# Expert tiles with the down product behind the next tile's up product, and all transposes in one place on 64 rows

## The reference

```python
def _moe2_ref(x, w_gate, w_local, w1, w2):          # x 4x576x512, w1 8x512x1024, w2 8x1024x512
    logits = np.einsum('bsd,de->bse', x, w_gate)
    local_gate = 1.0 / (1.0 + np.exp(-np.einsum('bsd,de->bse', x, w_local).squeeze(-1)))
    for b in range(B):
        prev_e = -1
        for s in range(S):
            fresh_e = int(np.argmax(logits[b, s]))
            e = fresh_e if (s == 0 or local_gate[b, s] < 0.5) else (prev_e if prev_e >= 0 else fresh_e)
            prev_e = e
            p = softmax(logits[b, s])
            h = np.maximum(x[b, s] @ w1[e], 0.0)
            out[b, s] = p[e] * (h @ w2[e])
```

## Time and profile before

| | us |
|---|---|
| median of 3 runs | 859.98 |
| lowest and highest | 859.12, 860.97 |
| the profiled execution: its time | 860.46 |
| its span between first and last record | 858.6 |
| PE busy (share of the span) | 841.0 (98%) |

### The profile page before, as it was taken

The page is one execution under the profiler, slowest core; times in us unless marked ns, Lnnn a source line. Parts: engine busy times, 40 slices in busy tenths (PEclk is TensorE's granted clock), DMA queues, the critical chain, the costliest instruction groups (busy, mean ns, idle before and its releaser), DMA issues.

```text
span 858.6 us, 19447 instructions
## 1 busy us (share of the span) xinstructions
PE 841.0 (98%) x7168; PEld 728.8 (85%) x7169; DVE 403.5 (47%) x730; ACT 340.7 (40%) x751; POOL 243.1 (28%) x286
## 2 busy tenths in 40 slices
PE   7899999999999999999999999999999999999996
PEld 6899999799999998799989989988778888888885
DVE  5677777511255245335536754543872432432221
ACT  4677777411145236215513522541432432522221
POOL 5977878793000000000000000039141112112111
PEclk9999999999999999999999999999999999999999
DMA  7454443139222012102201202415341341311111
GB/s 170 133 140 119 113 118 102 52 124 24 11 86 65 13 50 67 31 1 87 62 1 62 62 25 81 165 37 186 125 155 39 128 146 37 132 45 43 37 37 43
DMA packets 36088, 67.68 MB, mean 79 GB/s; under 512 B 11336, under 2 KB 11464, under 8 KB 36040
## 3 DMA queue, kind: packets, MB, share of 16 engines
q1 hardware_dynamic: 26168, 44.90, 19.7%
q10 hardware_dynamic: 6512, 11.64, 4.5%
q0 software_dynamic: 3360, 10.49, 3.8%
HBM read 57.58 MB, written 9.98 MB: 79 GB/s over the span
## 4 chain that ended last, share of the span: by engine, by line
PE 90%; DVE 3%; ACT 2%; POOL 2%; issue 1%; DMA 1%; ACTq 0%; POOLq 0%; DVEq 0%
PE bank L1700 23%; PE bank L1702 23%; PE bank L1701 23%; PE bank L1640 4%; PE bank L1585 4%; PE bank L1610 4%; PE bank L1893 2%; PE bank L1595 1%; PE bank L1747 1%; PE bank L1845 1%; DMA stage<-gate_rows 1%; DVE stage L1173 1%; PE bank L1573 1%; PE bank L1776 1%; PE bank L1626 1%
## 5 line engine op out<-in xcount | busy, mean ns | idle before, releaser
L1142 DVE SCALAR_TENSOR_TENSOR hid_lo<-bank,hid_hi 128x384 fp32r<-128x384 f32 x96 | 53.5, 557 | 210.1 <-ACT hid_hi L971 210.0
L1702 PE MATMUL bank<-uT_hi,W 128*128 128x384 f32 x384 | 129.8, 338 | 0.0
L1700 PE MATMUL bank<-uT_hi,W 128*128 128x384 f32 x384 | 129.6, 338 | 0.0
L1701 PE MATMUL bank<-uT_lo,W 128*128 128x384 f32 x384 | 129.1, 336 | 0.0
L971 ACT ACTIVATE hid_hi<-bank 128x384 fp32r<-128x384 f32 x96 | 46.9, 488 | 186.9 <-PE bank L1702 186.8
L995 ACT ACTIVATE stage<-stage 128x512 f32<-128x512 f32 x135 | 84.6, 627 | 77.0 <-DVE stage L1173 70.5
L1700 PE MATMUL bank<-W,hid_hi 128*128 128x512 f32 x288 | 114.0, 396 | 0.1
L1702 PE MATMUL bank<-W,hid_lo 128*128 128x512 f32 x288 | 113.8, 395 | 0.0
L1701 PE MATMUL bank<-W,hid_hi 128*128 128x512 f32 x288 | 113.6, 394 | 0.0
L1173 DVE TENSOR_TENSOR stage<-rows,stage 128x512 f32<-128x512 f32 x135 | 89.0, 687 | 10.7 <-ACT stage L995 8.5
L1404 DVE TENSOR_TENSOR hT_lo<-bank,hT_hi 128x512 fp32r<-128x512 f32 x40 | 27.6, 691 | 105.5 <-ACT hT_hi L1034 105.5
(11 more groups left out here) (287 smaller groups left out, 1528.9 us busy)
## 6 DMA issues: line engine op xcount, KB each, us to landing
rows<-in_moe_w SPq DMA_DIRECT2D x12, 1024.0 KB, 6.4
stage<-gate_rows ACTq DMA_DIRECT2D x38, 256.0 KB, 3.2
stage<-in_moe_w_ch SPq DMA_DIRECT2D x16, 512.0 KB, 3.8
qk_raw<-in_q SPq DMA_DIRECT2D x32, 144.0 KB, 3.6
vv<-in_v SPq DMA_DIRECT2D x32, 144.0 KB, 2.8
x_rows<-rows SPq DMA_DIRECT2D x6, 768.0 KB, 3.2
qk_raw<-in_k SPq DMA_DIRECT2D x30, 144.0 KB, 3.5
late_stage<-in_moe_w SPq DMA_DIRECT2D x4, 1024.0 KB, 6.6
```

Source lines behind the costliest of these rows:

```text
L1142: dve.scalar_tensor_tensor(out=hid_lo[:, n % 2], in0=bank[:, HB[n % 2], 0:TOK], scalar=0.0, in1=hid_hi[:, n % 2].bitcast(F32), op0=ALU.max ...
L1700: pe.matmul(dst, lhs_hi, rhs_hi, start=start, stop=False)
L1701: pe.matmul(dst, lhs_hi, rhs_lo, start=False, stop=False)
L1702: return pe.matmul(dst, lhs_lo, rhs_hi, start=False, stop=stop)
```

## The change

- **Order on PE.** A step of tile i is now: both up halves of tile i (24 matmuls), the whole down product of tile i - 1 (24 matmuls), then in one place the transposes of h of tile i, both halves, and of x of tile i + 2. The down product of the last tile stands alone behind the loop. In the written-out part the down product of tile 2 is cut: chunks 0 to 3 stand before the loop, 4 to 7 in step 3.
- **Transposes on 64 rows.** Each 128x128 transpose of the loop becomes two of 64 rows by 128 columns, one for each half of the tokens, which write to two banks (2 and 3, or 6 and 7). 24 instead of 12 per tile. In front of each group stands `settled(pe)`, a semaphore count of no other use.
- **A second transposed x.** `xT_hi_odd`, `xT_lo_odd` lie on memory of `rows`; the loop runs over pairs of tiles, even and odd. Tile i + 2 is transposed in step i, and tile i + 3 is gathered behind it; before it was i + 1 and i + 2.
- **ACT and DVE.** Splits of weights (both kinds) stand at the start of a step, ahead of the relus, and before they stood behind a tile's work, but for the case DOWN_NOW. `weigh(i - 1)` comes in step i, ahead of the low parts of h.

```diff
@@ the loop @@
         def expert_steps(eng, step):
             end = load_last(eng)
-            with eng.Fori(EARLY_T + 1, FULL) as i:
-                step(i)
-            with eng.Fori(FULL, TILES) as i:
-                with eng.If(end >= i):
-                    step(i)
+            step(EARLY_T + 1, 1)
+            with eng.Fori(EARLY_T // 2 + 1, FULL // 2) as n:
+                step(2 * n, 0)
+                step(2 * n + 1, 1)
+            with eng.Fori(FULL // 2, TILES // 2) as n:
+                for odd in range(2):
+                    with eng.If(end >= 2 * n + odd):
+                        step(2 * n + odd, odd)
             return end
@@ POOL @@
-            def step(i):
+            def step(i, par):
                 scatter(i - 1)
-                pool.wait_ge(xg_used, i + 2)
-                gather(i + 2)
+                pool.wait_ge(xg_used, i + 3)
+                gather(i + 3)
@@ POOL, before the loop @@
             scatter(0)
+            pool.wait_ge(xg_used, 3)
+            gather(4)
...
             scatter(1)
-            pool.wait_ge(xg_used, 4)
-            gather(4)
+            pool.wait_ge(xg_used, 5)
+            gather(5)
@@ ACT @@
+            def hT_halves(i, g):
+                act.wait_ge(tr_done, 2 * i + g + 1)
+                act.wait_ge(b_done, i)
+                if g == 1:
+                    act.wait_ge(xg_used, i + 3)
+                act.activation(by_half(hT_hi[:, 4 * g:4 * g + 4]), turned_half(g, H_COLS[g]), ACT.Copy)\
+                   .then_inc(hT_hi_out, 1)
-            def step(i):
+            def step(i, par):
                 todo = table(act, TODO, i, 7)
-                with act.If((todo & DOWN_NOW) != 0):
-                    prepare(i - 1, 1)
-                tile_work(i)
-                with act.If((todo & DOWN_LATER) != 0):
+                with act.If((todo & (DOWN_LATER | DOWN_NOW)) != 0):
                     prepare(i - 1, 1)
                 with act.If((todo & UP) != 0):
                     prepare(i, 0)
+                h_relu(i, 0)
+                h_relu(i, 1)
+                hT_halves(i, 0)
+                hT_halves(i, 1)
+                x_hi_halves(i + 2, par)
@@ DVE @@
-            def step(i):
+            def step(i, par):
                 todo = table(dve, TODO, i, 7)
-                with dve.If((todo & DOWN_NOW) != 0):
-                    prepare(i - 1, 1)
-                h_lo(i, 0)
-                h_lo(i, 1)
-                x_lo(i + 1)
-                with dve.If((todo & DOWN_LATER) != 0):
+                with dve.If((todo & (DOWN_LATER | DOWN_NOW)) != 0):
                     prepare(i - 1, 1)
                 with dve.If((todo & UP) != 0):
                     prepare(i, 0)
-                weigh(i)
+                weigh(i - 1)
+                h_lo_halves(i, 0)
+                h_lo_halves(i, 1)
+                x_lo_halves(i + 2, par)
@@ PE @@
+            def turn_h_halves(i, g):
+                if g == 0:
+                    pe.wait_ge(h_out, 2 * i + 2)
+                else:
+                    pe.wait_ge(xT_out, i + 2)
+                settled(pe)
+                for c in range(4):
+                    at = (4 * g + c) * P
+                    for half, rr in enumerate(HALVES):
+                        mm = pe.transpose(bank[:, TURNED[g], H_COLS[g]][:, half, c * HALF:c * HALF + HALF],
+                                          hrow[rr, at:at + P], ident[rr, rr])
+                mm.then_inc(tr_done, 1)
-            def step(i):
+            def step(i, x_par):
                 own_ = of_tile(i)
-                up_start(i, *own_)
-                up_rest(i, own_[0])
-                down_start(i, *own_)
-                turn_h(i, 1)
-                turn_x(i + 1)
-                down_part(i, own_[0], range(2, NEC))
+                up_start(i, *own_, x_par)
+                up_part(own_[0], 1, range(KC), x_par)
+                if isinstance(i, int):
+                    down_part(i - 1, 0, range(4, NEC))
+                else:
+                    down_start(i - 1, *of_tile(i - 1), range(NEC))
+                turn_h_halves(i, 0)
+                turn_h_halves(i, 1)
+                turn_x_halves(i + 2)
...
-            down_part(2, 0, range(2, NEC))
+            down_part(2, 0, range(2, 4))
+            turn_x_halves(4)
             pe.wait_ge(tables_ready, 1)
-            expert_steps(pe, step)
+            end = expert_steps(pe, step)
+            down_start(end, *of_tile(end), range(NEC))
```

More of the change, by code:

```diff
@@ L1074, in _ @@
             tile_work(2)
+            x_hi_halves(4, 0)
             act.wait_ge(tables_ready, 1)
@@ L1540, in _ @@
                 bank[:, 6, 0:3 * TP].rearrange("p (w i) -> p i w", w=3)[:, EARLY_T:TILES, :], ALU.add)
+            x_lo(3, 1)
             piece_lo(1, 1, 1)
-            weigh(2)
+            x_lo_halves(4, 0)
             piece_lo(1, 1, 2)
             piece_lo(1, 1, 3)
-            expert_steps(dve, step)
+            weigh(expert_steps(dve, step))
         @block.tensor
```

72 lines of the change are left out of this document (53 added, 19 removed).

## The result

The changed kernel takes 875.36 us (median of 4 runs, 874.56 to 876.27), the kernel before 859.90 beside it on the same chip: a ratio of 1.0182, with a 95% interval of 1.0167 to 1.0197. The prediction was 856.0 with 849.5 to 862.0 and the sign the other way. It was wrong.

The account below looks back on a forecast made before the run. PE was taken to bound the kernel. 17 steps at -0.33 us, +0.65 on the way in and +0.9 on the way out sum to -4.0: 856.4 profiled, 856.0 for the median, range 849.5 to 862.

Parts of the forecast that it names:

- What bounds the kernel: Expert tiles: PE is busy 12.49 of 12.50 us, so a step is as long as PE's row of instructions.
- The wait for relu goes: Transposes of h: they come a whole down product after relu, so PE's wait disappears, gaining 0.23 us a step.
- 24 transposes and the changes of shape, 0.87 + 0.36 us: Each step: 24 64-row transposes cost 0.87 us against 1.32 for twelve; two array shape changes add 0.15 and 0.21.
- Rival 4: Transposes: the 64-row halves don't run side by side, 0.072 us each, +14.6 - 4.0, time 870; 5%.
- Rival 1: Array shape changes are free, hidden by the queue behind a long product: gain 10.5 us, time about 849.5; 13%.
- The register load at the seam, taken at 0: Between steps: 48 queued instructions lasting 0.87 us hide the register load, 0.58 us on ACT, so it costs nothing.
- Rival 2: Seam between steps: register load and branches stand open behind short transposes, 0.58 us a step, +5.9, time 866; 10%.
- Rival 3: Costs eating the gain: part of the open seam or a drain per transpose group, 0.15 to 0.35 us a step; 16%.
- The way in, +0.65: Before the loop: one more group of x transposes, 0.29 us, and a pair of shape changes, 0.36, lost once.
- The way out, +0.9: Tile 19's last down product: nothing hides the turn of h, so PE waits 0.9 us once.
- rival 5: Gathered x lands beyond the slack in more than the two steps with weight loading: +2 us or more; 3%.

Follow-up runs that it names:

- e7: Changed kernel with the odd tile's register load moved ahead of the even tile's transposes, inside a loop pair only: 871.01 us.
- e16: e2 with the `settled` marks put back ahead of the transposes: 863.53 us.
- e3b: Changed kernel with the waits and marks of the three transpose groups moved ahead of the last six down products, transposes left in place: 874.80 us.
- e12: Changed kernel with e5, e6, e7 and tile 3's register loads moved ahead of the last part of tile 2's down product: 865.17 us.
- e6: Changed kernel with `gather(4)` moved back behind the mask `oh_p` on POOL, ahead of `scatter(1)`: 874.68 us.
- e5: Changed kernel with the last down product moved from behind the loop into the last tile's own branch: 871.37 us.
- e1: Changed kernel with all 24 transposes of a step moved ahead of the last six down products: 864.45 us.
- e11: e1 plus e5, e6, e7 and tile 3's register loads moved ahead of the last part of tile 2's down product: 860.45 us.
- e15: e2 with twelve unread pairs of 64-row transposes ahead of the last 128-row transpose in each looped step: 894.94 us.
- e2: Changed kernel with 12 transposes of 128 rows a step in the same place, without marks, instead of 24 on 64 rows: 863.39 us.
- e9: e2 with one unread pair of 64-row transposes ahead of the last 128-row transpose in each looped step: 869.25 us.
- e10: e2 plus e5, e6, e7 and tile 3's register loads moved ahead of the last part of tile 2's down product: 859.17 us.

## Why the prediction was wrong, point by point

- **What bounds the kernel** (PE, a step as long as its row of instructions) was right; every term that moved the time was idle time of PE.
- **The wait for relu goes**: right. No step of after waits for ACT.
- **24 transposes and the changes of shape, 0.87 + 0.36 us**: too dear by 0.25. With the load out of the way (e7) it is 0.32 + 0.89 us from the last product to the next, 0.98 more than the 0.227 of two products in a row. The transposes are 24 x 0.031 to 0.034 of that, and both changes together about 0.2: 0.09 on the way in where I took 0.15, and some 0.13 on the way out where I took 0.21. Rival 4 is out. Rival 1 is not right, as the changes do cost something, but its 0.87 us was nearer to the 0.98 than my 1.23.
- **The register load at the seam, taken at 0**: this is the step that failed. It said that 48 instructions lasting 0.87 us are queued ahead of the load, more than the 0.58 that it takes. The runs show both sides otherwise. When the load began in the pair, 23 of the 48 were left, 0.37 us of transposes; at the branch none was. And from its start to the next product it is 1.15 us: the load with its registers takes the 0.58, but the instructions of the next product stand behind it. So PE stood idle for 0.56 and 1.01 us. What is queued ahead shrinks in time when the instructions become short. The step is 12.91 us instead of 12.20, 0.71 more; as the last of the 17 has no seam behind it, this is 11.0 us in the table above.
- **Rival 2** had this very mechanism, with 0.24 us a step as the point from which it decides and 866 us in full; its price was ACT's 0.58. It was the case that came about, with 10%. Its size lacked the branch, which costs another 0.4 us each second time. It was read from a load on ACT, since none on PE stood open in the kernel before; but the rows of PE's sequencer in before had the length: the load of tile 4 begins at 650.00 and the last register instruction of the next product at 651.06, 1.1 us, hidden there behind six products of 0.227. Of the two figures of the Trainium skill that I named beside it, the register load's ("DMA: Bandwidth & Descriptors", Latency and other measured facts) agrees with the 0.58 us in the trace and the 0.62 that moving the load gained. The queue depth of 64 instructions ("TensorE: Matmul & The Clock Gate", the table at its head) would hide it, and did not: no seam's load had more than 34 instructions ahead of it.
- **Rival 3**, a drain at each of the three groups: the marks are worth 0.0 (e16) to 0.15 us (e3b) a step.
- **The way in, +0.65**: the terms counted were right in kind, but two were taken at 0 that weren't. `gather(4)` ahead of `oh_p` on POOL held DVE's `first` for 3.33 us and PE for 1.29; I had looked for who waits for `oh_p` on PE, not for who runs beside it. And two register loads stand open behind the x transposes for 1.36 us; moving them ahead gained 0.66 (e12 is at 637.53 - 618.15 = 19.38 where e6 had 20.04).
- **The way out, +0.9**: hT was there when forecast. In after DVE wrote its first low part by 856.8, T + 1.8 for T + 2.0 counted, and e5 waited 1.12 us. What I didn't see is that the last down product stands behind the skipped branches of six tiles and a load, 3 us more, and that the clock falls meanwhile, 1.7 us more.
- **x lands late**, rival 5: not in after; once in e1 (1.24 us) where the transposes stand 1.4 us earlier, and once in e11 (0.7).

The sum: 11.0 + 2.8 + 5.2 + 0.6 = 19.6 us more than forecast; the profiled execution took 875.92 us where the sum had come to 856.4.

## What to carry to other kernels

A register load or branch is hidden here by how long the last instructions ahead of it last, the 34 at most that the sequencer has passed on and PE hasn't begun. It is not hidden by how many there are in all, nor by how long the whole row is: 24 short transposes more (e15) hid nothing. Making those last instructions shorter can open it, so a load belongs behind the long products, ahead of a row of short ones. Its price is in the trace before anything is changed: the sequencer's own rows have its start, and the distance to the engine's next instruction can be compared with what is queued; a trace with the load moved is the test. When work is deferred by one turn of a loop, price the last turn by itself: what branches it skips, what wait it has no cover for, and what clock PE has behind that wait. And when an operation is moved on POOL, look at what DVE runs beside it, not only at who waits for it.

## What the runs showed of the hardware that I had not expected

- PE's sequencer needs 0.58 us for a register load with its check, 1.13 to 1.30 us from the load's start to the next product, and 0.4 more where the loop's branch stands ahead of it. It hid all of this behind 12 transposes of 128 rows (1.23 us), and not in full behind 24 on 64 rows (0.78 us). With pairs on 64 rows put ahead of the last transpose, the gap was 0 and 0 at one pair, 0 and 0.13 at four, 0.54 and 0.95 at eight, 0.46 and 0.88 at twelve.
- When such a load began, PE had 14 to 34 instructions (weight loads and matmuls) still to begin in the pair, and 0 to 30 at the branch, where the transposes stand behind all products.
- One pair of transposes on 64 rows between those of 128 costs 0.35 us, 0.06 of it for the transposes and the rest for two changes of shape.
- DVE's operation on 25 columns took 3.33 us instead of 0.84 while POOL issued an indirect DMA and ran three operations on 468 columns, 2.83 us together; with the same POOL operation but no gather ahead of it, 0.84. Which of the two held it, the runs don't tell apart, since only their order was changed.
- The clock went from 1.00 to 0.50 behind an idle time of PE of 4.16 us. In the first 2 us behind idle times of 1.77 (e11), 2.12 (e2) and 3.10 (e1) its mean was 0.55 to 0.65, and behind 2.13 (e16) 0.50. But behind 2.13 us in e9 it stayed at 1.00, as behind 0.73 (e10) and 1.12 (e5): idle times of the same length went both ways.
